# Feed-forward in three unrolled blocks of 512 tokens, part of the routing inside the last block, rows stored ahead of the last weight loads

## What is computed

```python
x = attention(q, k, v, proj)                 # (1536, 512)
h = x @ w_in                                 # w_in (512, 2048)
g = np.where(h > 0, h, np.exp(np.minimum(h, 0)) - 1)
y = g @ w_out                                # w_out (2048, 512)

out = y.copy()
c = (y @ w_skip) > 0                         # tokens that are computed further
logits = y[c] @ w_gate                       # 8 experts
e_idx = argmax(logits);  gate = softmax(logits)[e_idx]
for e in range(8):                           # w1 (8, 512, 1024), w2 (8, 1024, 512)
    out[c & e_idx == e] += gate * (relu(y @ w1[e]) @ w2[e])
```

## Time and profile before

| | |
|---|---|
| median of 3 runs | 696.99 us (695.63 to 697.05) |
| profiled execution, its own time | 697.44 us |
| its span, first to last instruction | 695.6 us |
| PE busy | 643.9 us, 93% of the span |
| DVE, ACT, POOL busy | 369.3, 326.2, 245.5 us |
| mean granted TensorE clock | 0.976 of full speed |

### The profile page before, as it was taken

The page is one execution under the profiler, slowest core; times in us unless marked ns, Lnnn a source line. Parts: engine busy times, 40 slices in busy tenths (PEclk is TensorE's granted clock), DMA queues, the critical chain, the costliest instruction groups (busy, mean ns, idle before and its releaser), DMA issues.

```text
span 695.6 us, 9823 instructions
## 1 busy us (share of the span) xinstructions
PE 643.9 (93%) x3632; PEld 593.1 (85%) x3632; DVE 369.3 (53%) x495; ACT 326.2 (47%) x505; POOL 245.5 (35%) x206
## 2 busy tenths in 40 slices
PE   3889999989999999999999999999999985999996
PEld 3688888888888888999999999999999965999995
DVE  6787777777777775356431223222322256556442
ACT  2366666766676668555443334233423330343330
POOL 5134476677776768804110012000004007412111
PEclk9699999999999999999999999999999986999999
DMA  7663464646464420452020002000356781999100
GB/s 169 148 135 84 106 159 115 161 113 147 114 155 126 102 70 17 144 159 91 1 91 1 1 0 90 0 0 0 116 214 244 245 318 57 317 381 329 73 11 25
DMA packets 67960, 84.00 MB, mean 121 GB/s; under 512 B 34260, under 2 KB 44500, under 8 KB 67920
## 3 DMA queue, kind: packets, MB, share of 16 engines
q1 hardware_dynamic: 66640, 79.83, 38.7%
q0 software_dynamic: 1280, 3.65, 1.6%
HBM read 56.64 MB, written 8.44 MB: 94 GB/s over the span
## 4 chain that ended last, share of the span: by engine, by line
PE 75%; DVE 11%; issue 5%; ACT 4%; DMA 3%; SPq 0%; POOL 0%; POOLq 0%; DVEq 0%; ACTq 0%
PE banks L1241 19%; PE banks L1252 19%; PE banks L1365 8%; PE banks L1380 6%; PE banks L1174 4%; DVE probs_lo L866 4%; PE banks L1205 3%; PE banks L1207 3%; PE banks L1206 3%; PE banks L1189 3%; PE banks L1190 3%; DVE k_hi_rows_T L835 2%; DVE q_hi_rows_T L835 2%; ACT o_and_den L690 2%; DMA y_rows<-y 2%
## 5 line engine op out<-in xcount | busy, mean ns | idle before, releaser
L1241 PE MATMUL banks<-x_hi,w_split 128*128 (+1 forms) x512 | 141.7, 337 | 0.0
L935 DVE SCALAR_TENSOR_TENSOR g<-exp_min_h,banks 128x384 f32<-128x384 f32 x64 | 35.5, 554 | 188.7 <-ACT exp_min_h L741 188.7
L512 POOL TENSOR_TENSOR probs_lo<-probs,probs_hi 128x768 fp32r<-128x768 f32 x64 | 107.7, 1695 | 68.0 <-ACT probs_hi L679 67.8
L1252 PE MATMUL banks<-w_split,g_hi 128*128 128x512 f32 x384 | 120.4, 394 | 0.1
L738 ACT ACTIVATE exp_min_h<-banks 128x384 f32<-128x384 f32 x64 | 31.5, 492 | 167.9 <-PE banks L1241 167.9
L671 ACT ACTIVATE probs<-banks 128x768 f32<-128x768 f32 x96 | 77.6, 809 | 67.3 <-PE banks L1190 67.3
L843 DVE TENSOR_REDUCE row_max<-banks 128x1 f32<-128x768 f32 x96 | 89.0, 951 | 28.8 <-PE banks L1174 28.7
L1241 PEld LDWEIGHTS banks<-x_hi,w_split 128*128 128x128 f32 x512 | 93.6, 188 | 2.7
L1241 PE MATMUL banks<-x_lo,w_split 128*128 (+1 forms) x256 | 86.0, 336 | 0.0
L1252 PEld LDWEIGHTS banks<-w_split,g_hi 128*128 128x128 f32 x384 | 70.6, 188 | 12.3 <-DVE g_lo L909 0.5
L679 ACT ACTIVATE probs_hi<-probs 128x768 fp32r<-128x768 f32 x96 | 80.6, 841 | 0.0
(11 more groups left out here) (163 smaller groups left out, 1030.4 us busy)
## 6 DMA issues: line engine op xcount, KB each, us to landing
expert_w<-in_moe_w SPq DMA_DIRECT2D x32, 1024.0 KB, 7.1
w_raw<-in_moe_w_in SPq DMA_DIRECT2D x16, 256.0 KB, 4.2
w_raw<-in_moe_w_out SPq DMA_DIRECT2D x16, 256.0 KB, 5.0
qk_nat<-in_q SPq DMA_DIRECT2D x16, 192.0 KB, 3.9
qk_nat<-in_k SPq DMA_DIRECT2D x16, 192.0 KB, 4.2
v_nat<-in_v SPq DMA_DIRECT2D x16, 192.0 KB, 3.9
q_hi_rows_T<-qk_hi_T SPq DMA_DIRECT2D x16, 192.0 KB, 2.8
k_hi_rows_T<-qk_hi_T SPq DMA_DIRECT2D x16, 192.0 KB, 3.1
```

The costliest lines, as they stand in the source:

```text
L512: pool.tensor_tensor(p_lo[:, n % RING, :, 0:HALF], probs[:, n % RING, :].rearrange("p (b n) -> p b n", b=2), p_hi[:, n % RING, :, 0:HALF]. ...
L1241: mm = pe.matmul(banks[:, j % 2, 0:BN], w, x, start=(c == 0 and w is hi and x is x_hi), stop=(c == KC - 1 and w is lo))
L1252: mm = pe.matmul(banks[:, 2 + t, :], g, W[:, j, part, :], start=(j == 0 and i == 0), stop=(j == FT - 1 and i == 2))
```

## The change

The feed-forward gets BLOCKS = 3 blocks of BN = 512 tokens (BT = 4 tiles), all written out with no hardware loop. Matmuls of `up` have 512 columns, `down` uses four banks (2 to 5) and 12 matmuls. The places for `gh` and `gl` go from four to three. One tile is transposed per step, in steps 3 to 6 of the next block, through bank 6. The routing is cut in two parts: tiles 0 to 7 are chosen, ranked and placed during steps 9 to 14 of the last block (`choose(0)`, `ranks(0)`, `places(0)`, `gates(0)`, `slots(0, ...)`), tiles 8 to 11 after it. The last two downs are issued tile by tile, with transposes and scores between. SP stores `y_rows` ahead of `out` for the last block, both ahead of the last four weight pieces (expert 3), which wait for the gather of expert 0. POOL waits for `y_rows` alone before the gathers.

```diff
-BLOCKS, BT = 4, 3
+BLOCKS, BT = 3, 4
...
-        gh = sb("g_hi", [P, 4, BN], F32R)[0]
-        gl = sb("g_lo", [P, 4, BN], F32R)[0]
+        gh = sb("g_hi", [P, 3, BN], F32R)[0]
+        gl = sb("g_lo", [P, 3, BN], F32R)[0]
...
-            for j in range(FT):
-                sp.wait_ge(s_["y_step"], 18 * (BLOCKS - 1) + (j + 1 if j < FT - 1 else 18))
+            def early_expert(j):
+                sp.wait_ge(s_["y_step"], (FT + BT - 1) * (BLOCKS - 1) + j + 1)
                 load_expert(j // 4, j % 4)
-            store_y(BLOCKS - 1)
+
+            for j in range(12):
+                early_expert(j)
+            store_y(BLOCKS - 1, y_rows, "y_kept")
+            store_y(BLOCKS - 1, out, "y_stored")
+            sp.wait_ge(gathered[0], 16)
+            for j in range(12, FT):
+                load_expert(j // 4, j % 4)
...
             normalise(PAIRS - 2, *low_ready(QT * HEADS - 1))
-            split_x(1)
-            normalise(PAIRS - 1, s_["x_ready"], 2)
+            normalise(PAIRS - 1, s_["xt_step"], 2 * PAIRS - 2)
+            split_x(1, slice(0, 2))
+            split_x(1, slice(2, 4))
...
             pool.wait_ge(e_loaded[0], 64)
+            pool.wait_ge(s_["h_done"], FT * BLOCKS)
             split_first(0)
 
             pool.wait_ge(s_["idx_ready"], 1)
-            pool.wait_ge(s_["y_stored"], 1 + 32 * BLOCKS)
+            pool.wait_ge(s_["y_kept"], 32 * BLOCKS)
...
+            def slots(i, a):
+
+                for t in range(parts[i].start, parts[i].stop):
+                    if a == 0:
+                        pe.wait_ge(s_["onehot_ready"], t + i + 2)
+                    mm = pe.matmul(ps_slots[:, a, :], onehot[:, t, :], told[:, t, :, 3 * a:3 * a + 3], start=False,
+                                   stop=(t == TILES - 1), skip_group_check=True)
+                return mm
+
+            for n in range(BLOCKS):
+                last = n == BLOCKS - 1
                 pe.wait_ge(s_["x_ready"], n + 1)
                 for j in range(FT):
                     up(n, j)
...
+                    if n and 3 <= j < 3 + BT:
+                        y_transposes(BT * (n - 1) + j - 3)
+                    if n and 4 <= j < 4 + BT:
+                        scores_of(BT * (n - 1) + j - 4)
+                    if last and j == 10:
+                        ranks(0)
+                    elif last and j == 13:
+                        slots(0, 0)
+                    elif last and j == 14:
+                        pe.wait_ge(s_["told_gates"], 1)
+                        slots(0, 1)
                     if j >= 2:
                         down(n, j - 2)
...
+            last_down(0)
+            last_down(1)
+            y_transposes(EARLY_T)
+            last_down(2)
+            y_transposes(EARLY_T + 1)
+            scores_of(EARLY_T)
+            last_down(3)
+            y_transposes(EARLY_T + 2)
+            scores_of(EARLY_T + 1)
+            y_transposes(EARLY_T + 3)
+            scores_of(EARLY_T + 2)
+            scores_of(EARLY_T + 3)
+
+            ranks(1)
```

More of the change, by code:

```diff
@@ L969, in _ @@
[L969 to L972 removed]
+                dve.tensor_copy(lg_flat[:, n * n9:n * n9 + n9], banks[:, 7, 0:n9]).then_inc(s_["lg_read"], 1)
             count = [0]
@@ new lines, in places @@
+            def places(i):
+                t = parts[i]
+                dve.wait_ge(s_["rank_done"], i + 1)
+                link(dve.tensor_tensor(mix[:, t, :], ps_rank[:, t, :], chosen_b[:, t, :], ALU.mult))
+                link(dve.tensor_reduce(dest[:, t], mix[:, t, :], AX.X, ALU.add))
+                for n in range(t.start, t.stop):
+                    dve.tensor_scalar(onehot[:, n, :], slot_no[:, :], dest[:, n:n + 1], None, ALU.is_equal)\
+                        .then_inc(s_["onehot_ready"], 1)
@@ L1025, in _ @@
+            g_low(FT * BLOCKS - 1)
+            for i in range(EARLY_T, TILES):
+                y_T_copy(i)
+            logits_copy(BLOCKS - 1)
+            choose(1)
+            places(1)
+            lg, best = logits[:, :, 0:EXPERTS], pick_e[:, :, 0:EXPERTS]
             dve.wait_ge(s_["slots_done"], 1)
-            told_slot = banks[:, 7, 0:2 * EXPERTS * 3].rearrange("p (a e i) -> p a e i", a=2, i=3)
+            told_slot = ps_slots.rearrange("p a (e i) -> p a e i", i=3)
             link(dve.tensor_copy(slot[:, :, 0:3], told_slot[:, 0, :, :]))
@@ L1243, in up, with down_tile @@
-                mm.then_inc(s_["h_done"], 1)
+                    hi, lo = (W[:, j, i, c * P:c * P + P] for i in range(2))
+                    x_hi, x_low = xh[:, n % 2, c, :], x_lo[:, c, part]
+                    for i, (w, x) in enumerate(((hi, x_hi), (hi, x_low), (lo, x_hi))):
+                        mm = pe.matmul(banks[:, g % 2, 0:BN], w, x, start=(c == 0 and i == 0),
+                                       stop=(c == KC - 1 and i == 2))
+                mm.then_inc(s_["h_done"], 1)
+            def down_tile(n, j, t):
+                at = (n * FT + j) % 3
+                hi, lo = (x[:, at, t * P:t * P + P] for x in (gh, gl))
+                for i, (g, part) in enumerate(((hi, 2), (hi, 3), (lo, 2))):
+                    mm = pe.matmul(banks[:, 2 + t, :], g, W[:, j, part, :], start=(j == 0 and i == 0),
+                                   stop=(j == FT - 1 and i == 2))
+                return mm
@@ L1245, in down @@
             def down(n, j):
-                pe.wait_ge(s_["gl_ready"], n * FT + (j + 1))
-                if not isinstance(n, int) and j == 0:
+                pe.wait_ge(s_["gl_ready"], n * FT + j + 1)
+                if n and j == 0:
                     pe.wait_ge(s_["y_ready"], n * BT)
                 for t in range(BT):
-                    hi, lo = (x[:, j % 4, t * P:t * P + P] for x in (gh, gl))
-                    for i, (g, part) in enumerate(((hi, 2), (hi, 3), (lo, 2))):
-                        mm = pe.matmul(banks[:, 2 + t, :], g, W[:, j, part, :], start=(j == 0 and i == 0),
-                                       stop=(j == FT - 1 and i == 2))
+                    mm = down_tile(n, j, t)
@@ L1329, in _ @@
                                stop=(t == TILES - 1))
             mm.then_inc(s_["counted"], 1)
-            pe.wait_ge(s_["lg_read"], 1 + BLOCKS)
-            for t in range(TILES):
-                pe.wait_ge(s_["onehot_ready"], t + 2)
-                mm = pe.matmul(banks[:, 7, 0:EXPERTS * 3], onehot[:, t, :],
-                               told[:, t, :, 0:3], start=(t == 0), stop=(t == TILES - 1))
-            mm.then_inc(s_["slots_done"], 1)
-            pe.wait_ge(s_["told_gates"], 1)
+            slots(1, 0).then_inc(s_["slots_done"], 1)
@@ L1340, in _ @@
+            pe.wait_ge(s_["told_gates"], 2)
             pe.wait_ge(s_["idx_ready"], 1)
-            for t in range(TILES):
-                mm = pe.matmul(banks[:, 7, EXPERTS * 3:2 * EXPERTS * 3], onehot[:, t, :],
-                               told[:, t, :, 3:6], start=(t == 0), stop=(t == TILES - 1), skip_group_check=True)
-            mm.then_inc(s_["gates_done"], 1)
+            slots(1, 1).then_inc(s_["gates_done"], 1)
             def rows_T(e):
```

420 lines of the change are left out of this document (207 added, 213 removed).

## The result

The changed kernel takes 688.83 us, median of 4 runs (688.47 to 689.57). The kernel before took 697.02 beside it (695.63 to 697.79). The profiled execution took 688.83, its span is 686.6 where it was 695.6.

What follows compares the result with a forecast made beforehand. Bound by PE through the feed-forward, then by the store of y and the gather before expert 0. Terms -4.6 + 1.5 = -3.1 took the profiled 697.44 to 694.3, or 693.9 us against the median 696.99; range 691.6 to 696.6.

Steps and rivals of the forecast that it cites:

- the sizes in the feed-forward on PE: Feed-forward steps on PE: 268.0 us before, 267.5 after at 0.232 a matmul, a gain of 0.5.
- writing out the loop: Feed-forward blocks: replacing the hardware loop by written-out code gains 0 and costs nothing.
- no wait inside the steps: Feed-forward steps: the longer ACT and DVE operations hold PE nowhere, cost 0, with slack of a microsecond or so.
- no wait at the start: First up of the feed-forward: POOL's split of x stays 0.4 us ahead of PE, cost taken as 0.
- routing in the last block: Ranks and slots of the early tiles on PE's path in the last block: +1.5 us, bounds 0.7 and 2.5.
- Tail: Last downs to the logits on PE, four tiles woven in: gain 0.6 us, only the last scores waiting 0.1 to 0.2.
- routing behind the logits: From the copy of the logits to the gather's index: 3.8 us left with four tiles, 5.92 + 0.17 before.
- the store hidden: Store of y's last rows: lands 3.3 to 4.8 us later, by 570.5, hidden behind the index with 1.9 to spare.
- Covered by 1.1: Between gather 0 and expert 0: DVE's gate work, about 4.6 us, is ready 1.1 us before the transposed rows need copying.
- The wait at gather 1: Ahead of expert 1: its gathered rows land at 589.2, wanted at 587.7, so PE waits +1.5 us, bounds 0 and 4.5.
- gather 1 is in time: Rival: sharing DMA engines in turns, expert 1's rows land at 586.7, ahead of 587.7; 692.4 us, chance 0.25.
- My sign for a wrong prediction: Ahead of expert 1's rows: the prediction counts as wrong if, among other signs, PE does not stop there.

Runs made afterwards that it cites:

- e3: The changed kernel with the last four weight pieces again ahead of the two stores of y, without waiting for a gather; 691.49 us.
- e1: The changed kernel with GpSimd's second split of expert 0's w2 right behind its first, ahead of the gathers; 687.74 us.
- e5: The changed kernel with gathers 0 and 1 ahead of GpSimd's second split, last gates behind expert 0's transposed rows, DVE's counts in expert 2; 685.62 us.
- e10: The changed kernel with only gathers 0 and 1 issued ahead of GpSimd's second split, VectorE's order kept; 688.40 us.
- e7: The kernel before with only the last block's stores moved ahead of the last four weight loads, which wait for the first gather; 697.52 us, ratio 1.0007.
- e8: The changed kernel with the routing of the eight early tiles moved back behind the last block; 695.29 us.
- e2: The changed kernel with the last four tiles' gates behind expert 0's transposed rows on DVE, their slots behind its first product on PE; 688.55 us.
- e9: e6 with 19 instead of 15 unread matmuls behind the slots and 3 more behind the transposes of expert 0's rows; 685.42 us.
- e11: e9 with DVE's low part of expert 1's weights moved behind the low parts of expert 0's hidden values; 685.05 us.
- e6: e5 with 22 unread matmuls of 512 columns added where PE waits between the logits and expert 0; 684.93 us.

## Why the prediction was wrong

**Failed: the sizes in the feed-forward on PE.** "The change has 48 steps of 24 matmuls of 512 columns; at the 0.232 of down that is 48 x 5.57 = 267.5." The mechanism was right (fewer matmuls, the same columns), the price of one was not. It is 0.2267, so the term is -6.9, not -0.5, and 6.4 us off. That is more than the whole miss of 5.1; the terms below together take a little of it back. Of the gain, 768 ups of 0.1753 against 576 of 0.2267 make -4.0, and 0.045 less in each of 64 downs -2.9. The trace of before has two places with 512 columns alone. In the feed-forward it is the row of downs behind the last up: from 561.75 to 563.11 six of them start, 0.2267 apart, behind others at 0.23. The experts' second products have 24 in a row. In the chain of before:

```profile
605.77 5.49 PE banks L1380 x24
```

That is 0.2288 each. The price was to be had there to within 1%, and I did not look.

**Right, by the traces:** writing out the loop costs and gives nothing; no wait inside the steps; no wait at the start. No run takes the loop or the ring of three alone.

**Right, sizes a little off:** routing in the last block (+1.5, came +1.2: 0.41 for ranks, twice 0.21 for slots, and about 0.12 on each of three downs behind them).

**Tail: "only the last scores wait, 0.1 to 0.2" failed by about 1 us.** Between the end of the last up (547.63) and the logits lie 36 downs of 0.2267, and four tiles of 0.44 and 0.79, 13.1 us of work in 14.37. PE waits twice for DVE's low part, 0.2 each time. The second low part takes 1.02 instead of 0.69, beside GpSimd's first split, which the change placed there. The scores at the end wait for DVE's copies of y: the last 16 matmuls take 1.94, where two tiles of 0.79 make 1.58. The granted clock fell to 0.50 at 561.6, ahead of the copy of the logits; in the kernel before it fell at 569.3, a microsecond behind it.

**Right:** routing behind the logits, 3.73 us for my 3.8, and the store hidden (landed 2.7 after its issue). GpSimd's start was 0.30 after the index instead of 0.9: I had read 0.9 off a wait for a DMA, and it holds for that (0.88 in e3) and not for a wait for DVE. With the logits 6.6 earlier than forecast (562.00 for 568.6), gather 0 started at 566.03 and not near 573.3.

**Failed: "Covered by 1.1."** I took DVE's gate work at its old length, "about the same 4.6 in sum". It ran beside an idle GpSimd before; the change starts the gather early and so moves GpSimd's split beside it. That is the new wait, +3.0 and with it a longer stretch of expert 0's product at the low clock, +0.6. About 0.6 of the gates' delay is the one operation beside the issue of gather 0. e1, e5 and e10 took it away or part of it, e7 and e8 made it where it had not been or longer. I had looked at what DVE does, not at who works next to it.

**The wait at gather 1** (+1.5) did not come, and neither did rival "gather 1 is in time" describe why. The transfer was as slow as I had said (7.9 for my 6.7, start 9.25 behind gather 0 for my 9.17). PE was later than I had said. With the gates out of the way it came at 1.99 (e2). My sign for a wrong prediction, that PE does not stop ahead of expert 1's rows, was met.

The Trainium skill, "SBUF — State Buffer", section "Who interferes with whom", states that VectorE and GpSimd share a second pair of SBUF ports as a lock: casts, copies and tensor_scalar in the two-port modes, and VectorE operations with two SBUF inputs, wait for a GpSimd operation that holds it, reductions don't. The traces agree: casts, tensor_scalar and two-input operations of 0.17 that start beside the split last until GpSimd's operation ends (up to 1.25), and the reduction and the reciprocal keep 0.18. I had not weighed this page against the change, and it is the rule that spoke against it.

## What to carry over

Read the price of a matmul of one width from a stretch in which only that width runs; a 2% error of it is worth more than every wait around it when a thousand of them follow. When a change takes a wait away, list the engines that newly work side by side: here the wait had kept GpSimd idle while VectorE did its smallest operations. And expect a second wait close behind the first: of the 4.8 us that the earlier store freed, 2.7 arrived, and they came back only when gates, gathers and splits were ordered together (e5, 3.2 us below the changed kernel).

## What the runs showed of the hardware

A 512-column matmul directly in a row with others takes 226.7 ns, one of 384 columns 175.3, each with its weight load; 12 of 512 behind 12 of 384 take 2.76 instead of 2.72, and 2.84 to 2.88 behind transposes and scores. The Trainium skill, "TensorE: Matmul & The Clock Gate", section "Back-to-back issue gap", gives 216 ns for one of 512 by itself, without the load, and 131 ns for a stream with loads; the rows show 11 ns more than the first, and the second nowhere.

GpSimd's gather starts 0.30 us after VectorE's index is written and 0.88 to 0.89 after a store has landed (e3 and the kernel before).

A VectorE operation of four elements a partition, 0.17 to 0.19 alone, can last 1.1 us beside GpSimd's split. Side by side with GpSimd's issue of a gather most keep 0.16 to 0.24 (e1). Not all do beside the last gather ahead of a split: one took 0.74 in the changed kernel and one 0.66 in e10 (567.90), each ending within 0.05 of the issue's end. With another gather next, the operation of 0.74 took 0.17 (e5, e10). What makes the difference, no run shows.

Where unread matmuls filled PE's waits up to expert 0, TensorE's clock stood at 2.4 GHz from 564.9 (e9) or 566.1 (e11) on, and expert 0's product took 7.2 and 7.4 us instead of 9.0. The six ahead of the ranks met the upper level in e6 and the lower one in e9, where it had fallen at 561.5, before they began (561.70); in e11 it fell at 562.7, just behind the start of the first (562.56). What decided that, no run here shows.
